# Moving three pieces of work in a fused attention and MLP kernel: the uniform value to ScalarE, low parts to GpSimd, block moves to SyncE

## The reference

```python
# attention: 4 batches, 8 heads, 576 positions, head size 64
scores = scale * np.matmul(q, k.transpose(0, 1, 3, 2))
thresh = np.max(scores, axis=-1, keepdims=True) - tau
scores = np.where(scores >= thresh, scores, -1000000000.0)
scores = scores - np.max(scores, axis=-1, keepdims=True)
attn = np.exp(scores)
attn = attn / (np.sum(attn, axis=-1, keepdims=True) + 1e-09)
x = np.matmul(attn, v)                      # then 2304 tokens x 512
# first MLP, 512 -> 2048 -> 512
h = x @ w_in
x = (np.maximum(h, 0.0) + alpha * np.minimum(h, 0.0)) @ w_out
# second MLP, 512 -> 1024 -> 1024 -> 512
out = (((x @ w1) * (x @ w2)) @ w3) @ w_out2
```

## Time and profile before

| | |
|---|---|
| Time, median of 3 runs | 1096.91 us (1095.68 to 1100.75) |
| Profiled execution, its own time | 1102.26 us |
| Its span in the profile | 1100.4 us |
| Busy: TensorE, VectorE | 1007.5 us (92%), 528.5 us (48%) |
| Busy: ScalarE, GpSimd | 417.7 us (38%), 454.6 us (41%) |
| SyncE's queue (q1), ScalarE's queue (q10) | 130.45 MB, 24.78 MB |

### The profile page before, as it was taken

One profiled execution on the slowest core, in us unless ns is written; L12 is line 12 of the kernel. 1 busy time (PEld: TensorE's weight loads), 2 busy tenths in 40 slices (PEclk: granted clock), 3 DMA queues, 4 the chain that ended last, 5 costly groups with the idle time before them and its releaser, 6 DMA issues.

```text
span 1100.4 us, 18074 instructions
## 1 busy us (share of the span) xinstructions
PE 1007.5 (92%) x6848; PEld 914.1 (83%) x6848; DVE 528.5 (48%) x1388; ACT 417.7 (38%) x1002; POOL 454.6 (41%) x565
## 2 busy tenths in 40 slices
PE   3799967898999798979999999999999999999998
PEld 2566644777777676858999999999999999999998
DVE  5999897878888887941233222222211111111111
ACT  5566565555555554522333333333212112111211
POOL 5766566655565564511334444444321112112111
PEclk9999976999999999999999999999999999999999
DMA  5588888686776757474442333436310111011000
GB/s 172 151 237 246 246 245 269 174 233 179 200 201 172 223 144 219 102 218 127 153 139 85 128 127 133 151 142 280 129 66 23 65 66 44 23 66 43 23 22 23
DMA packets 51623, 156.38 MB, mean 142 GB/s; under 512 B 8144, under 2 KB 19408, under 8 KB 47312
## 3 DMA queue, kind: packets, MB, share of 16 engines
q1 hardware_dynamic: 41936, 130.45, 36.9%
q10 hardware_dynamic: 9600, 24.78, 8.6%
HBM read 80.22 MB, written 32.51 MB: 102 GB/s over the span
## 4 chain that ended last, share of the span: by engine, by line
PE 59%; DVE 14%; DMA 9%; ACT 7%; issue 4%; POOL 4%; ACTq 3%; SPq 1%; POOLq 0%
PE psum L627 19%; PE psum L659 19%; PE psum L613 10%; DMA zbuf<-ybuf 6%; DVE nmx L845 5%; PE psum L573 4%; DVE e_ring L852 4%; PE psum L538 3%; ACTq L745 3%; ACT e_ring L718 3%; PE psum L586 2%; POOL g L966 2%; DVE g_raw L889 2%; PE psum L521 2%; ACT g_raw L753 1%
## 5 line engine op out<-in xcount | busy, mean ns | idle before, releaser
L966 POOL TENSOR_TENSOR g<-g_raw,g 128x288 fp32r<-128x288 f32 x192 | 157.8, 826 | 388.2 <-ACT g L830 235.0
L659 PE MATMUL psum<-xy,w_a 128*128 128x288 f32 x1536 | 206.1, 295 | 0.6 <-DVE y_buf L950 0.6
L659 PEld LDWEIGHTS psum<-xy,w_a 128*128 128x128 f32 x1536 | 205.2, 188 | 0.8 <-DVE y_buf L950 0.8
L521 PE MATMUL psum<-ks,qs 128*128 128x288 f32 x640 | 125.0, 327 | 44.0 <-DVE e_ring L852 32.4
L994 POOL TENSOR_SCALAR e_ring<-e_ring,rden,uni 128x576 f32<-128x576 f32 x144 | 121.7, 846 | 79.5 <-DVE rden L868 71.4
L521 PEld LDWEIGHTS psum<-ks,qs 128*128 128x128 f32 x640 | 105.1, 211 | 59.1 <-DVE e_ring L852 38.9
L852 DVE SCALAR_TENSOR_TENSOR e_ring<-psum,thr,e_ring 128x576 f32<-128x576 f32 x144 | 117.3, 815 | 37.6 <-ACT e_ring L718 37.2
L889 DVE SCALAR_TENSOR_TENSOR g_raw<-g_raw,beta_sb,psum 128x288 f32<-128x288 f32 x128 | 65.2, 514 | 132.2 <-ACT g_raw L753 131.5
L538 PE MATMUL psum<-zbuf,vs 128*64 128x320 f32 (+1 forms) x640 | 110.8, 443 | 15.5 <-DMA zbuf<-ybuf 14.8
L845 DVE TENSOR_REDUCE nmx<-psum 128x1 f32<-128x576 f32 x144 | 107.9, 750 | 18.5 <-PE psum L521 18.2
L827 ACT COPY g_raw<-psum 128x288 f32<-128x288 f32 x64 | 25.6, 400 | 236.1 <-PE psum L659 236.1
(11 more groups left out here) (54 smaller groups left out, 1109.9 us busy)
## 6 DMA issues: line engine op xcount, KB each, us to landing
xy<-xs SPq DMA_DIRECT2D x16, 1152.0 KB, 6.0
raw_w<-weights SPq DMA_DIRECT2D x52, 256.0 KB, 4.1
zbuf<-ybuf SPq DMA_DIRECT2D x64, 180.0 KB, 3.6
zbuf<-ybuf ACTq DMA_DIRECT2D x64, 180.0 KB, 5.4
k_raw<-k SPq DMA_DIRECT2D x16, 576.0 KB, 7.4
q_raw<-q SPq DMA_DIRECT2D x16, 576.0 KB, 7.2
zbuf<-ybuf SPq DMA_DIRECT2D x64, 144.0 KB, 3.6
zbuf<-ybuf ACTq DMA_DIRECT2D x64, 144.0 KB, 4.9
```

What stands on the lines that cost most here:

```text
L521: last = mm(dst, qs[:, par, at:at + P], ks[:, par, part, h, cols], start=(m == 0), stop=(m == 2 * len(terms) - 1))
L659: last = mm(psum[:, 2 * ab + f % 2, 0:CH], w_a[:, wp, slot, (f % 4) * P:(f % 4 + 1) * P], xy[c][:, xp, kt, :], start=(n == 0), stop=(n == ...
L966: sub = lambda out_, a, hi: nc.gpsimd.tensor_tensor(out_, a, hi.bitcast(F32), ALU.subtract)
```

## The change

Three things are moved. The uniform value is made on ScalarE, as Relu(1/576 - sum/576) of the masked row's sum, with a constant tile `share` of 1/576 that GpSimd writes once at the start. The sum of a row in which anything passes is at least one, so the Relu gives zero there. The low parts of all early pieces are made on GpSimd, in the piece's own step. And SyncE issues six block moves in each of its two steps; ScalarE issues one in each of its four.

```diff
--- before.py
+++ after.py
@@ -203,6 +203,7 @@
         g_raw = sb("g_raw", [RAW, CH])
 
         warm = sb("warm", [2], F32, attn)
+        share = sb("share", [1], F32, attn)
         tau_sb = sb("tau_sb", [1], F32, attn)
         q_raw = sb("q_raw", [2, SEQ], F32, attn)
         k_raw = sb("k_raw", [2, SEQ], F32, attn)
@@ -394,6 +395,9 @@
                 for k in range(QD):
                     dst, src = move(n, 2 * y, (2 * y + k) % QD)
                     sp.dma_start(dst, src).then_inc(s_z[y], 16)
+                    if k % 2 == 1:
+                        dst, src = move(n, 2 * y + 1, (2 * y + 3 + k // 2) % QD)
+                        sp.dma_start(dst, src).then_inc(s_z[y], 16)
 
             def load_early(j):
                 if j >= 4:
@@ -703,6 +707,15 @@
                     act.wait_ge(s_wc_out[i % 2], 16 * (i // 2))
                 copy(w_c_part(i, 0), product_bank(i)).then_inc(s_wph, 1)
 
+            def uniform_of(t):
+
+                i = t % TILES
+                act.wait_ge(s_mask, t + 1)
+                if t == 0:
+                    act.wait_ge(s_warm, 1)
+                nc.scalar.activation(uni[:, i:i + 1], den[:, i:i + 1], ACT.Relu, bias=share[:, 0:1], scale=-1.0 / SEQ)\
+                    .then_inc(s_uni, 1)
+
             def threshold_of(t):
                 i = t % TILES
                 act.wait_ge(s_max, t + 1)
@@ -740,9 +753,8 @@
                 act.wait_ge(s_t, TILES * (n + 1))
                 if n >= 1:
                     act.wait_ge(s_pv[y], n)
-                for k in (2 * half, 2 * half + 1):
-                    dst, src = move(n, 2 * y + 1, (2 * y + 1 + k) % QD)
-                    act.dma_start(dst, src).then_inc(s_z[y], 16)
+                dst, src = move(n, 2 * y + 1, (2 * y + 1 + half) % QD)
+                act.dma_start(dst, src).then_inc(s_z[y], 16)
 
             def negative_of(cc, f, h):
                 act.wait_ge(s_h, FT * cc + (f + 1))
@@ -778,6 +790,8 @@
                         for m in range(2):
                             act.wait_ge(s_wc_out[m], 16 * FT // 2)
                     negative_of(ck, f, fbank(f))
+                if tile_at(s, 1) is not None:
+                    uniform_of(tile_at(s, 1))
                 if tile_at(s) is not None:
                     threshold_of(tile_at(s))
                     exp_of(tile_at(s))
@@ -857,11 +871,6 @@
                 dve.wait_ge(s_mask, t + 1)
                 nc.vector.tensor_scalar(den_eps[:, i:i + 1], den[:, i:i + 1], 1e-9, None, ALU.add).then_inc(s_eps, 1)
 
-            def uniform_of(t):
-                i = t % TILES
-                nc.vector.tensor_scalar(uni[:, i:i + 1], nmx[:, i:i + 1], thr[:, i:i + 1], 1.0 / SEQ,
-                                        ALU.is_gt, ALU.mult).then_inc(s_uni, 1)
-
             def reciprocal_of(t):
                 i = t % TILES
                 dve.wait_ge(s_eps, t + 1)
@@ -888,9 +897,9 @@
                 raw = g_raw[:, raw_h(f), :]
                 nc.vector.scalar_tensor_tensor(raw, raw, beta_sb[:, a:a + 1], h, ALU.mult, ALU.add).then_inc(s_g, 1)
 
-            def piece_lo(dst_lo, dst_hi, j, raw=None):
+            def piece_lo(dst_lo, dst_hi, j):
                 dve.wait_ge(s_w_hi, 2 * j + 2)
-                sub(dst_lo, raw_w[:, 1, :] if raw is None else raw, dst_hi).then_inc(s_w_lo[1], 1)
+                sub(dst_lo, raw_w[:, 1, :], dst_hi).then_inc(s_w_lo[1], 1)
 
             for s in range(STEPS):
                 if s == 2:
@@ -903,7 +912,6 @@
                     dve.wait_ge(s_beta, 1)
                 if tile_at(s, 1) is not None:
                     mask_of(tile_at(s, 1))
-                    uniform_of(tile_at(s, 1))
                 for ck, f in hidden_done(s - 1):
                     activation_of(ck, f, 0, fbank(f))
                 if tile_at(s) is not None:
@@ -917,10 +925,6 @@
                 for part in range(X_PARTS):
                     if pair_at(s, LAG_X[part // 2]) is not None:
                         x_lo(pair_at(s, LAG_X[part // 2]), part)
-                j = piece_at(s - 1)
-                if j is not None and j % 2 == 1:
-                    slot = early_slot(j)
-                    piece_lo(w_a[:, 1, slot, :], w_a[:, 0, slot, :], j // 2, early_raw(j))
                 i = product_made(s - 2)
                 if i is not None:
                     dve.wait_ge(s_wph, i + 1)
@@ -964,6 +968,7 @@
         @block.gpsimd
         def _(pool):
             sub = lambda out_, a, hi: nc.gpsimd.tensor_tensor(out_, a, hi.bitcast(F32), ALU.subtract)
+            nc.gpsimd.memset(share[:, :], 1.0 / SEQ)
             nc.gpsimd.memset(warm[:, :], 0.0).then_inc(s_warm, 1)
 
             def split_kq_lo(n, lows, t):
@@ -982,9 +987,14 @@
                 if lows and lows[-1] >= 4:
                     pool.wait_ge(s_kq_lo, LO_PARTS * n + lows[-1] + 1)
 
-            def piece_lo(dst_lo, dst_hi, j, raw=None):
+            def early_lo(j):
+                slot = early_slot(j)
+                pool.wait_ge(s_w_hi, j + 1)
+                sub(w_a[:, 1, slot, :], early_raw(j), w_a[:, 0, slot, :]).then_inc(s_w_lo[j % 2], 1)
+
+            def piece_lo(dst_lo, dst_hi, j):
                 pool.wait_ge(s_w_hi, 2 * j + 1)
-                sub(dst_lo, raw_w[:, 0, :] if raw is None else raw, dst_hi).then_inc(s_w_lo[0], 1)
+                sub(dst_lo, raw_w[:, 0, :], dst_hi).then_inc(s_w_lo[0], 1)
 
             def probs_of(t):
                 i = t % TILES
@@ -1004,10 +1014,8 @@
                 split_kq_lo(*parts_at(s, LO_STEPS, LO_PARTS), tile_at(s, 2))
                 for ck, f in hidden_done(s - 1):
                     activation_lo(ck, f)
-                j = piece_at(s)
-                if j is not None and j % 2 == 0:
-                    slot = early_slot(j)
-                    piece_lo(w_a[:, 1, slot, :], w_a[:, 0, slot, :], j // 2, early_raw(j))
+                if piece_at(s) is not None:
+                    early_lo(piece_at(s))
 
             for c in range(2):
                 for f in range(FT):
```

## The result

The changed kernel takes 1083.44 us in the median of 4 runs (1082.45 to 1087.95), the kernel before 1098.83 beside it (4 runs, 1095.68 to 1102.62). The ratio is 0.9867 with a 95% interval of 0.9821 to 0.9912, so 14.6 us less, with 9.7 to 19.7 in the interval. The profiled execution took 1082.92 us, with a span of 1081.0; its counterpart of before had a span of 1100.4. That one is near the top of its kernel's runs (3.4 us above the median of 32 later ones, with a mean granted clock of 0.972 where theirs is 0.9775 in the median), so the difference of the two spans, 19.4, is some 3 to 5 us more than the medians give.

The account below looks back on a forecast made before the run. Bound taken: the attention loop of mask, maximum and exponential through VectorE and ScalarE, 2.61 us a step. 9.9 - 2 + 5.5 + 7 - 1.6 = 18.8 off 1096.91 gives 1078, rounded to 1080; range 1070 to 1093.

Parts of the forecast that it names:

- signs of being wrong: Waits for chunk load or keys appear, SP's 12 issues take over 11 us, or attention steps stay at 2.61.
- Uniform value (9.9 - 2): Attention loop: 76 steps each 0.13 us shorter save 9.9; the added ScalarE activation costs 2 in late steps.
- the upper of the two ends: Saving per attention step from the removed VectorE instruction: 0.13 us, against 0.06 if the accumulator read fills the slot.
- The price of 2: ScalarE's added activation costs 2 us, of up to 3.6, in the 18 steps in which ScalarE was late.
- Low parts (+5.5): Twenty low parts leave VectorE for GpSimd: 1.5 us won between 144 and 186, 4 from ten others, 5.5 in sum.
- the bound of 2 lost: Between 18 and 40 us GpSimd becomes the limit: nothing won, at worst 2 us lost.
- Block moves (+7): ScalarE's queue: fewer moves land sooner; at most TensorE's 14.8 us of waits go, half taken, as the chunk load is next.
- The weight loads' part, -1.6: Weight stretch: two more moves ahead of a piece's load, 0.82 us each, cost 1.6 us in ScalarE's wait.
- The rule on issuing engines: All issues share 16 DMA engines, so spreading saves only issue time: the moves' 7 would be near 1, time about 1087.
- Keys ("still hidden, with 1.2 us left"): Keys issued up to 3.3 us later on SP still land before ScalarE reads them, with 1.2 us left.
- rival 3: SP issues over 0.92 us make keys late in 14 pairs; at 1.1, 31 us lost, 1111; chance 0.08.
- Rivals 1, 2 and 4: Low vector saving, moves hidden anyway: 1090 (0.14); GpSimd bounds piece stretches: 1089 (0.10); change does nothing: 1097 (0.08).

Follow-up runs that it names:

- e1_uniform: The kernel before with only the uniform value moved from VectorE to ScalarE; 1099.26 us, ratio 1.0006.
- e9_moves_uniform: The kernel before with the block moves and the uniform value changed, low parts of odd pieces still on VectorE; 1085.5 us, ratio 0.9893.
- e3_moves: The kernel before with only the block moves shifted (SyncE 12, ScalarE 4); 1093.04 us, ratio 0.9943.
- e6_keys: The changed kernel with the keys' load one step earlier, ahead of the second half's moves; 1082.86 us, ratio 0.9841 to the kernel before.
- e11_store_first: The changed kernel with only the stores of x put ahead of the moves of their step; 1083.91 us, ratio 0.9864 to the kernel before.
- e7_both: The changed kernel with x stores and keys ahead of the second half's moves, odd chunk loads four steps earlier; 1073.16 us, ratio 0.9761 to the kernel before.

## Why the prediction was right, and which of its steps were not

1080 was forecast, and the medians are 1083.44 and 1083.86. The sum was 18.8 us and the forecast 16.9 below 1096.91; the comparisons gave 14.6 and 16.5. The number was right in part by luck. U was put at 9.9 - 2 = 7.9 and gave 3.0 to 5.5 when it was added to kernels with the moves, nothing elsewhere. M was put at 7 - 1.6 = 5.4 and gave 11.0 to 12.9 when it was added last. One was too high and the other too low. And of the prediction's own signs of being wrong two came: waits for the chunk load appeared and those for keys grew, and the twelve issues took 11.3 us at the pair shown. The other signs came as written (the step, the order on ScalarE, GpSimd above 85% and the most used engine from 144 to 186, the waits for moved blocks, the later stages).

- **Uniform value (9.9 - 2).** The step was read rightly: 2.48, and the upper of the two ends, since the accumulator read holds no slot. So was the count. In four pairs of traces that differ in U alone, 66 to 79 of the 143 intervals between masks are 0.10 to 0.15 us shorter, 7.9 to 9.5 us in sum; the two traces of the changed kernel itself have no such interval. The price of 2 is near, too: 1.5 at the late steps of `e1_uniform`. The wrong step is that 76 steps of 0.13 reach the time whole. They do not: between the traces with M and L the shortened intervals give 9.5 us, the last mask comes only 2.6 earlier, and the medians give 3.0 to 4.9; alone, U gives nothing (-0.7). The other intervals grew by the rest. Why they take back all of it without the moves and about half or more with them stays open.
- **Low parts (+5.5).** 4.9 alone, 2.8 to 5.3 on top of others: right, and also by place. From 18 to 40 GpSimd is busy 96% of the time. The changed kernel reaches the mask of step 19 at 42.13, and `e9_moves_uniform`, whose VectorE still has half the low parts, at 40.36: nearly the bound of 2 lost, not the value 0. Without U it goes the other way (42.81 before, 41.82 with L), so 0 is fair as a mean. From step 55 to 73, with a piece in most steps, L wins: 64.8 us with it in the changed kernel, 67.6 in `e9_moves_uniform`, and 1.9 to 2.4 us in the three other pairs of traces. 1.5 was forecast there.
- **Block moves (+7).** 6.3 alone was nearly the figure; on top of U it was too small by half. Of its working, "at most 14.8 us of waits go" came true wholly, and "what is late next is the chunk load" too, but its size was too small: 16.4 us of waits for the chunk stand against 14.8 removed. What the moves gave all the same lies elsewhere, by the table of stretches: 4.5 to 6.5 us before step 55, and 3.4 to 7.2 behind the last mask, where the last pair's blocks have nothing left to hide behind. The sum had neither. It treated the 14.8 us as if a wait removed were time gained, less the chunk's. The weight loads' part, -1.6, is right as a wait (ScalarE's waits for pieces are 6.4 + 4.3 = 10.7 us, where they were 5.2 + 4.3 = 9.5) and low as a price: the stretch from step 55 to 73 is 2.0 to 4.6 us longer with the moves in all four pairs.
- **The rule on issuing engines** (the Trainium skill, "DMA: Bandwidth & Descriptors", section "Issuing engines are not separate DMA queues"), by which the term would be near 1: `e3_moves` measured 6.3 (3.5 to 9.0), and the 14.8 us of waits went to none. That is not against the rule itself, which grants the saving of issue time; it is against the step from it to a price near 1. Issue time was not small here: ScalarE lost 33.1 us between its instructions before and 5.3 after. The gain can be in what stood ahead of a transfer on its issuing engine and in what the issues held up on ScalarE; how much was each, no run here separates. (By the forecast's own figures a term of 1 gives 1086, not 1087.)
- **Keys ("still hidden, with 1.2 us left").** This step is wrong. It took 0.82 us for each of the twelve issues; they took 0.94 at the pair shown, within rival 3's 0.92 to 1.02, and the stores of x behind them took 2.86 where they had taken 1.92. So the keys were issued 14.25 us after the first move instead of 8.59: 5.7 later, not 3.3. They landed faster than the 7.4 taken, and ScalarE waited 1.28 us for them, at 350.43. In all ScalarE waited 19.2 us in ten places, where it had waited 5.7 in two. Where rival 3 was wrong is the price: it made each such wait a loss of the pair, and `e6_keys` took 13 us of these waits away for 1.0 us that can't be told from none. The reason given against the rival, that an engine that issues alone has less to contend with, did not hold: with more of the issues on SyncE, each took longer (0.89 against 0.76 us in the mean of nine pairs).
- **Rivals 1, 2 and 4** fall with the figures above: the moves were not hidden, GpSimd cost some 2 us in one stretch of two traces, and not 10, and the time moved.

The largest thing that was missed is not in the sum at all: the chunk's wait was named as next and then left at half the term. The odd chunks' loads issued four steps earlier, the first diff above, are worth 8 to 10 us (0.9850 or 0.9867 against 0.9777). Side by side with `e11_store_first` it is 10.6 (1083.91 to 1073.28).

## What to carry to other kernels

When a queue gets more transfers, list everything that stands behind them and write beside each the time of its landing and of its first use, with the issue time that the busier queue may have and not the present one; the one with the least left is the next wait, and moving it ahead can be worth nearly as much as the change (here 8 to 12 us beside 15). A step that is made shorter may pay nothing, though the trace shows it shorter at every place: count it as a bound, and price it together with the transfers. Look at what stands behind the last tile, where nothing hides a late transfer. And a wait in the trace is no price: 13 us of ScalarE's waits for keys could go for nothing, while 11 us less of TensorE's waits for chunks went with 12 us less time, and in `e7_both` 13 us of waits for moved blocks came back beside a time that stayed. Before two single traces are compared, look at the granted clock and the busy time of both.

## What the runs showed of the hardware

- Twelve DMA issues of SyncE in a row took 0.94 us each (11.3 in all) at the pair shown, where eight had taken 0.82 each; in the mean of nine pairs it is 0.89 and 0.76. The single issues in the rows above go up to 1.43 us.
- ScalarE loses time of its own to the transfers that it issues: 33.1 us of idle time at its issues in the first 490 us with eight moves a pair, 5.3 with four.
- The record of VectorE's accumulator read (0.08 us) costs nothing: with the small instruction gone, the next one starts at the same time as that read.
- GpSimd's subtraction of 128 x 512 values took 1276 to 1292 ns in the means of twenty when VectorE had none of them (four kernels), and 1345 to 1405 in the means of ten when VectorE had as many (four kernels). Why, no run here shows.
- Parts of a change that are each tried alone may mislead: -0.1, 0.45 and 0.57% alone made 1.33 to 1.50% together.
